# Last two tiles of a mixture-of-experts layer outside the loop, their logits placed on chip

## Chip, cores, metric

One core of a Trainium2 chip. The metric is the device time of one execution in microseconds (us), lower is better.

## What is computed

Sliding-window attention over 4 x 768 tokens (8 heads of 64), then two layers of experts over the same 3,072 rows of 512 numbers. Both have 8 experts, each a 512 x 1024 and a 1024 x 512 matrix. They differ in who goes where:

```python
# first layer: each token to its own best expert
logits = x @ w_gate + modality_bias[modality_id]
e_idx = np.argmax(logits, axis=1)
h = np.maximum(x[mask] @ w1[e], 0.0)
out[mask] = gate_w[mask, None] * (h @ w2[e])
# second layer: greedy over all (token, expert) pairs, 384 tokens an expert
order = np.argsort(-(x @ w_gate).flatten())
...
if assigned[tok] >= 0 or counts[e] >= cap: continue
```

So the second layer can assign nothing before the logits of all 3,072 rows of the first layer's output are known.

## The kernel before

**First layer.** The tokens are sorted by expert into tiles of 128, at least 24 and at most `MAXT` = 31 of them; how many there are is known only on the chip. DVE (VectorE) computes tables in `build_slots` (line 1296): `idx`, the token of each place of each tile; `tab`, per tile its group (`T_GRP`), the parity of its weight buffer (`T_PAR`), whether weights are to be split at it (`T_SPLIT`), and the number of tiles less 3 (`T_N`). `table_ready` releases SP's, ScalarE's and TensorE's weight work.

Each tile runs through these steps, written out as a queue by hand on each engine:

- GpSimd `gather` (576): the rows of x of tile i, by indirect DMA, into `xg`; `scatter` (585): `y` with its 8 logits back to `y_rows` in memory (columns 512 to 519 are the logits). There is one `y`; it is written again only when its scatter has landed.
- TensorE `step1(i)` (817): `up(i)` half 0 (12 matmuls), `transpose_h(i-1)` (8 transposes), `up(i)` half 1 (12), `transpose_x(i+1)` (4), `down(i-1)` (24 matmuls, into bank 5).
- ScalarE `step` (1073): `h_hi(i-1)` (copies the transposed hidden values rounded, in two halves, into `hh`), two `relu(i)`, `x_hi(i+1)`.
- VectorE `step` (1406): `h_lo(i-1)` (line 1393, two halves: the rest that the rounding left, into `hl`), logits 5 to 7 of tile i-2, `x_lo(i+1)`, then, when `down(i-1)` is done, `y` (line 1418), two copies of gates, logits 0 to 4 of tile i-1 (line 1404, `second_logits`). `down(i)` on TensorE waits for `h_lo(i)`. Each value times weight product is three matmuls (high by high, high by low, low by high).

Tiles 0 to 2 are written out. Then each engine has a loop of `MAXT - 3` = 28 turns, with a condition inside: turn k does tile k + 3, if k is below the number of tiles less 3; `split_next(i)` behind a tile reads `T_SPLIT` from `tab` (lines 1094, 1446). The unused turns come last. Behind the loop stand the last `transpose_h` and `down`, the last `y`, its 8 logits and the last two scatters.

```python
with dve.Fori(0, MAXT - 3) as k:          # 1462
    with dve.If(k < tiles.k):             # 1463
        i = Index(k, 3)
        step(0, i)
        split_next(i)
step(0, tiles, cur=False)
```

**Between the layers.** SP waits until all scatters have landed and loads the 3,072 x 8 logits into `l2` (lines 471, 472): 24 columns of tokens on 128 partitions. VectorE fills small tiles meanwhile (1475 to 1494) and waits for `l2_loaded`.

**Second layer.** Rounds `ph` = 0 to 6 each find the expert that fills first: a radix search for a threshold, 8 steps t of 4 bits. In a step VectorE compares (`compare`, 1511, operations `ge`), TensorE counts (848), VectorE marks full experts (1529), TensorE spreads (853), VectorE takes the digit (`next_digit`, 1532). At t = 1 and 2 `finite` (1483) changes thresholds that would be read as NaN or infinity: three chained VectorE operations. From round 1 on, TensorE's matmuls of the experts already filled (`hidden` 889, `outward` 902) stand between the steps of the search, and VectorE's low parts too; `pick_early` (1625) and GpSimd's `pick_late` build the list of an expert's rows, which `gather_second` reads from `y_rows`.

**Attention** comes first; GpSimd prepares keys there (`key_spans`, 511) and constants, and stores 128 zero rows behind x (571).

Of the kernel before, what the change touches and what calls it, by code (L numbers as in the profile page):

```python
# [15 lines left out]
P = 128  # L16
# [11 lines left out]
TC = N // P  # L28
# [30 lines left out]
SOON = 5  # L59
# [45 lines left out]
def val(x):  # L105

    if not isinstance(x, Index):
        return x
    k = x.k if x.m == 1 else x.k * x.m
    return k + x.c if x.c else k  # L110


def two_layers_of_experts(nc, queries, k, v_win, modality_id, w_gate, modality_bias, w1, w2,
                          w_gate2, w1b, w2b, out):
    ctx = ExitStack()
    with ctx:
# [35 lines left out]
        tab = sb("tab", [P, 6, 32], I32)  # L152
        T_PAR, T_GRP, T_SPLIT, T_EID, T_N = range(5)
# [4 lines left out]
        gidx = sb("gidx", [P, 1], I32)  # L158
        sidx = sb("sidx", [P, 1], I32)
        eids = sb("eids", [P, E], I32)  # L160
# [12 lines left out]
        first.close()  # L173

        second = ExitStack()
        sc = lambda name, shape, dt=F32: second.enter_context(nc.sbuf_tensor(name, shape, dt))
        xh2 = sc("xh2", [P, KC, CAP], F32R)
        xl2 = sc("xl2", [P, KC, CAP], F32R)
# [181 lines left out]
        down_done, y_done = two("down_done"), two("y_done")  # L360
        gate_loaded, l2_out = sem("gate_loaded"), sem("l2_out")
        l2_loaded = sem("l2_loaded")
        dve_chain2 = sem("dve_chain2")
# [124 lines left out]
        def _(pool):  # L488
# [81 lines left out]
            g.nop().then_inc(const_ready, 1)  # L570
            pool.dma_start(x_d[N:N + P, :], zrow[:, :]).then_inc(pad_stored, 16)
            for m in range(3, B * HP):
                key_spans(m)
                spread_means(m)
# [9 lines left out]

            def scatter(st, i):
# [6 lines left out]
                pool.indirect_dma_start(out=dst[:, :], out_offset=bass.IndirectOffsetOnAxis(ap=sidx[:, 0:1], axis=0),  # L592
                                        in_=y[:, 0:w], in_offset=None).then_inc(scattered[st], 16)

            for stored in x_stored:
                pool.wait_ge(stored, 16 * (B + 1))
            pool.wait_ge(pad_stored, 16)
            pool.wait_ge(idx_ready, 1)
            gather(0, 0)
# [5 lines left out]
            tiles = Index(pool.value_load(tab[0:1, T_N, 0:1], min_val=NT - 3, max_val=MAXT - 3), 3)  # L605
            with pool.Fori(0, MAXT - 3) as k:
                with pool.If(k < tiles.k):
# [4 lines left out]
            chain.start(base + 2 * (tiles - 3))  # L612
            scatter(0, tiles - 2)
            scatter(0, tiles - 1)
            base = base + 2 * tiles - 4
            def gather_second(r, t):
# [37 lines left out]
        def _(pe):  # L654
# [117 lines left out]

            def product(ps, lhs, rhs, n):

                for c in range(n):
                    for t, (a, b) in enumerate(((0, 0), (0, 1), (1, 0))):
                        last = mm(ps, lhs[a][:, c, :], rhs[b](c), start=c == 0 and t == 0, stop=c == n - 1 and t == 2)  # L777
                return last

# [24 lines left out]

            def down(st, i, g, par):
                pe.wait_ge(hlo_done[st], val(2 * i + 2))
                pe.wait_ge(wlo_done[st], val((W1U + W2U) * (g + 1)))
                pe.wait_ge(y_done[st], val(i))
                s_ = bass.ds(par, 1) if not isinstance(par, int) else slice(par, par + 1)
                rhs = [lambda c, w=w: w[:, s_, c, :].rearrange("p o f -> p (o f)") for w in (w2h, w2l)]  # L810
                product(bank[5][:, :], (hh, hl), rhs, FC).then_inc(down_done[st], 1)

# [24 lines left out]
            tiles = Index(pe.value_load(tab[0:1, T_N, 0:1], min_val=NT - 3, max_val=MAXT - 3), 3)  # L837
            with pe.Fori(0, MAXT - 3) as k:
                with pe.If(k < tiles.k):
                    step1(Index(k, 3))  # L840
            step1(tiles, cur=False)


            def count(ph, t):
# [130 lines left out]
        def _(act):  # L975
# [132 lines left out]
            tiles = Index(act.value_load(tab[0:1, T_N, 0:1], min_val=NT - 3, max_val=MAXT - 3), 3)  # L1108
            with act.Fori(0, MAXT - 3) as k:
                with act.If(k < tiles.k):  # L1110
                    i = Index(k, 3)
                    step(0, i)
                    split_next(i)
            step(0, tiles, cur=False)

# [50 lines left out]
        def _(dve):  # L1166
# [129 lines left out]
            def build_slots(st):  # L1296
# [40 lines left out]
                if st == 0:  # L1337
# [57 lines left out]

            def second_logits(i, experts):
                if 0 in experts:
                    dve.wait_ge(y_done[0], val(i + 1))
                for e in experts:
                    if e >= 2:  # L1400
                        dve.wait_ge(l2_out, val(E * i + (e - 1)))
                    elif not isinstance(i, int) or i > 0:
                        dve.wait_ge(l2_out, val(E * i + (e - 1)))
                    stt(bank[6 + e % 2][:, :], y[:, 0:DM], 1.0, wg2[:, e, :], ALU.mult, ALU.mult, accum_out=y[:, DM + e:DM + e + 1]).then_inc(l2_out, 1)  # L1404

# [55 lines left out]
            tiles = Index(dve.value_load(tab[0:1, T_N, 0:1], min_val=NT - 3, max_val=MAXT - 3), 3)  # L1461
            with dve.Fori(0, MAXT - 3) as k:
                with dve.If(k < tiles.k):
                    i = Index(k, 3)
# [5 lines left out]
            base = base + 2 * (tiles - 3)  # L1470
            chain.start(base)


            chain = Chain(dve, dve_chain2)
            chain(vec.memset(owner[:, :], -1.0))
# [17 lines left out]
            for t in range(STEPS - 1, 3, -1):  # L1493
                chain(tt(digits[:, t, :], digits[:, t, :], digits[:, t - 1, :], ALU.bitwise_xor))
            dve.wait_ge(l2_loaded, 16)

            def prepare(ph):
# [13 lines left out]
            def compare(ph, t):  # L1511
                if t in (1, 2):
                    finite(thr[:, :])
# [243 lines left out]
```

## Time and profile before

| | |
|---|---|
| runs shown, us | 1064.84, 1066.01, 1074.94; median 1066.01 |
| profiled execution, us | 1066.68 (its span 1064.9) |
| granted TensorE clock, mean | 0.925 |
| TensorE busy | 84% of the span |
| attention | 0 to about 218 us |
| tables | to 242 us |
| first layer | 242 to 597 us |
| scatter, reload | to 604 us |
| second layer | 604 to 1065 us |

The profile is of one execution. PE is TensorE, DVE VectorE, ACT ScalarE, POOL GpSimd; a `q` behind a name (DVEq, PEldq) marks what the engine's sequencer does itself: register operations, loads of a register, branches. In brackets stands the engine's idle time before an instruction and what ended it; "issue" is idle time in which it waited for nothing that the profile shows. `x13` is the number of instructions in a row. Line numbers are those of the kernel before.

### The profile page before, as it was taken

The numbers are of one execution on the slowest core, as the hardware profiler recorded it, in microseconds if no ns is written. First come the engines' busy times: TensorE is split into PE (matmuls) and PEld (weight loads), VectorE is DVE, ScalarE is ACT, GpSimd is POOL, SyncE is SP. The second block draws the span as 40 slices with busy tenths as digits, with TensorE's granted clock in tenths as the row PEclk, the third lists the DMA queues.
The fourth block names the chain that finished last, engine by engine and source line by source line (L and its number), as shares of the span: only waits on it lengthen the run. The fifth ranks groups of instructions, "written<-read, shape, count | busy, mean of one in ns | idle before, by whom it ended". The sixth has DMA issues, their size and how long they took to land.

```text
span 1064.9 us, 21948 instructions
## 1 busy us (share of the span) xinstructions
PE 898.2 (84%) x7342; PEld 733.7 (69%) x7343; DVE 681.6 (64%) x1998; ACT 305.5 (29%) x626; POOL 285.1 (27%) x390
## 2 busy tenths in 40 slices
PE   4899999915899999999996233999898989998995
PEld 3787878714688888888885122868686867687884
DVE  5757576575666666666665567777777768674440
ACT  2544454505322212222221003223232322223330
POOL 5733344101012111111220005050515151414501
PEclk9999999956899999999998655999999999999998
DMA  9676675915011111111110123414141414155100
GB/s 195 122 160 135 133 153 100 280 50 185 11 51 40 50 40 40 40 40 40 40 50 20 24 71 119 159 51 169 50 169 54 165 61 159 61 204 172 32 29 30
DMA packets 45631, 99.94 MB, mean 94 GB/s; under 512 B 6736, under 2 KB 19072, under 8 KB 45440
## 3 DMA queue, kind: packets, MB, share of 16 engines
q1 hardware_dynamic: 26816, 61.63, 19.8%
q0 software_dynamic: 8064, 26.46, 7.9%
q10 hardware_dynamic: 10688, 11.01, 4.9%
q8 instruction: 39, 0.64, 0.2%
q14 instruction: 24, 0.20, 0.1%
HBM read 79.57 MB, written 19.51 MB: 93 GB/s over the span
## 4 chain that ended last, share of the span: by engine, by line
PE 69%; DVE 18%; issue 4%; POOL 3%; ACT 2%; DMA 2%; DVEq 0%; ACTq 0%; SPq 0%; POOLq 0%
PE bank L777 27%; PE bank L898 11%; PE bank L912 9%; PE bank L689 4%; PE bank L670 3%; PE bank L848 3%; DVE w_low L1649 2%; PE bank L730 2%; PE bank L707 2%; PE bank L801 2%; PE bank L679 2%; POOL slot_hot L635 2%; DVE xl L1653 1%; DVE ge L1517 1%; ACT xh L1042 1%
## 5 line engine op out<-in xcount | busy, mean ns | idle before, releaser
L1404 DVE SCALAR_TENSOR_TENSOR bank<-y,wg 128x512 f32<-128x512 f32 x200 | 132.0, 723 | 2.9
L635 POOL TENSOR_SCALAR slot_hot<-iota_l,mlo 128x128 bf16<-128x128 f32 x96 | 72.0, 766 | 214.7 <-DVE mlo L1622 214.7
L898 PE MATMUL bank<-xh,w_high 128*128 128x384 f32 x256 | 94.3, 368 | 16.1 <-DVE hl L1639 8.9
L777 PE MATMUL bank<-w_high,hh 128*128 x200 | 83.2, 416 | 13.2 <-DVE hl L1393 13.2
L777 PE MATMUL bank<-w_high,xh 128*128 x200 | 82.7, 414 | 10.7 <-DVE gates L1386 10.7
L592 POOL DMA_INDIRECT y_rows<-y,sidx x25 | 25.0, 998 | 243.2 <-DVE bank L1404 243.2
L898 PE MATMUL bank<-xh,w_low 128*128 128x384 f32 x256 | 88.1, 344 | 0.0
L898 PE MATMUL bank<-xl,w_high 128*128 128x384 f32 x256 | 87.9, 344 | 0.0
L1042 ACT ACTIVATE hh<-bank 128x512 fp32r<-128x512 f32 x50 | 27.1, 595 | 203.1 <-PE bank L801 203.1
L1418 DVE TENSOR_SCALAR y<-bank,gates 128x512 f32<-128x512 f32 x25 | 18.8, 751 | 101.1 <-PE bank L777 101.1
L912 PE MATMUL bank<-w_high,hh 128*128 128x512 f32 x192 | 82.3, 429 | 0.0
L1042 ACT ACTIVATE w_high<-w_landed 128x1024 fp32r<-128x1024 f32 x64 | 63.1, 1049 | 66.0 <-DMA w_landed<-in_moe_w 66.0
L777 PE MATMUL bank<-w_low,hh 128*128 x200 | 80.5, 403 | 0.0
L777 PE MATMUL bank<-w_high,hl 128*128 x200 | 80.3, 402 | 0.0
L777 PE MATMUL bank<-w_low,xh 128*128 x200 | 80.3, 402 | 0.0
L777 PE MATMUL bank<-w_high,xl 128*128 x200 | 80.2, 401 | 0.0
L1649 DVE TENSOR_TENSOR w_low<-w_landed,w_high 128x1024 fp32r<-128x1024 f32 x64 | 77.8, 1219 | 0.8
L848 PE MATMUL bank<-ge,cb 128*8 128x16 bf16 x1344 | 42.3, 170 | 41.7 <-DVE ge L1517 41.6
L912 PE MATMUL bank<-w_high,hl 128*128 128x512 f32 x192 | 75.7, 394 | 0.0
L912 PE MATMUL bank<-w_low,hh 128*128 128x512 f32 x192 | 75.5, 393 | 0.0
L848 PEld LDWEIGHTS bank<-ge,cb 128*8 128x8 bf16 x1344 | 36.2, 83 | 54.6 <-DVE ge L1517 50.8
L1118 ACT ACTIVATE hh<-bank 128x384 fp32r<-128x384 f32 x64 | 31.5, 492 | 140.2 <-PE bank L898 140.2
(285 smaller groups left out, 1932.5 us busy)
## 6 DMA issues: line engine op xcount, KB each, us to landing
w_landed<-in_moe_w SPq DMA_DIRECT2D x16, 2048.0 KB, 10.5
va<-in_v_win SPq DMA_DIRECT2D x16, 585.0 KB, 6.4
raw_w<-in_moe_w SPq DMA_DIRECT2D x4, 2048.0 KB, 11.3
k_raw<-in_k SPq DMA_DIRECT2D x16, 384.0 KB, 9.1
q_eye<-in_q ACTq DMA_DIRECT2D x16, 384.0 KB, 7.4
x_rows<-x ACTq DMA_DIRECT2D x12, 384.0 KB, 10.2
wg<-in_moe_w_gate SPq DMA_DIRECT2D x1, 2048.0 KB, 25.8
x_rows<-x SPq DMA_DIRECT2D x4, 387.0 KB, 7.2
```

Of the source, the lines that this page charges most:

```text
L592: pool.indirect_dma_start(out=dst[:, :], out_offset=bass.IndirectOffsetOnAxis(ap=sidx[:, 0:1], axis=0), in_=y[:, 0:w], in_offset=None).the ...
L635: last = g.tensor_scalar(slot_hot[:, j, :], iota_l[:, :], mlo[:, j:j + 1], None, ALU.is_equal)
L670: last = mm(bank[n % 2][QB * s_:QB * s_ + QB, PW * (2 * t + h):PW * (2 * t + h) + PW], qe[hp % 2][:, h, QB * j:QB * j + QB], kbt[hp % 2][: ...
L689: last = mm(bank[4 + (n + 1) % 2][WK:PW, MEAN0:MEAN0 + 2 * D], average[:, j, :], va[m % HP][0:WK, :, j, 0:D], start=j == 0, stop=j == NQ - 1)
L777: last = mm(ps, lhs[a][:, c, :], rhs[b](c), start=c == 0 and t == 0, stop=c == n - 1 and t == 2)
L848: last = mm(bank[7][0:E, 0:KSEARCH], cb[:, j, :], ge[:, j, :], start=j == 0, stop=j == TC - 1)
L898: last = mm(bank[fc % 2][:, 0:CAP], w[:, q % 2, c, f], a[:, c, :], start=c == 0 and t == 0, stop=c == KC - 1 and t == 2)
L912: last = mm(bank[2 + t % 2][:, :], a[:, c, rows], w[:, q % 2, c, :], start=c == 0 and n == 0, stop=c == FC - 1 and n == 2)
L1042: copy = lambda o, a: nc.scalar.activation(o, a, ACT.Copy)
L1118: nc.scalar.activation(hh2[:, fc, :], bank[fc % 2][:, 0:CAP], ACT.Relu).then_inc(hhigh_done, 1)
L1404: stt(bank[6 + e % 2][:, :], y[:, 0:DM], 1.0, wg2[:, e, :], ALU.mult, ALU.mult, accum_out=y[:, DM + e:DM + e + 1]).then_inc(l2_out, 1)
L1649: tt(low, whole, high.bitcast(F32), ALU.subtract).then_inc(low_done, 1)
```

## The change

1. A table row `T_TURN` gives each loop turn its tile: `max(0, k + tiles - MAXT)`. The loops have `MAXT - 4` = 27 turns, the unused ones come first, and a used turn reads its tile's number from the table. They now end with the last tile but one.
2. The end is written out on each engine. TensorE computes `down` of the last tile but one in two halves with `transpose_h` of the last between them, and `down` of the last into bank 4. ScalarE instead of VectorE writes the last two y, one of them into `y_last`.
3. SP loads `l2` when all but the last two tiles are stored. GpSimd has stored zeros in the logit columns in attention. The last two scatters wait for this load.
4. The logits of the last two tiles go into `l2` on chip: GpSimd makes two one-hots for each tile from its token numbers (`slot_lo` by partition, `slot_hi` by column), VectorE multiplies the logits with `slot_hi` (`placed`), two fp32 matmuls with `slot_lo` put them on their partitions (bank 5), VectorE adds them to `l2`.
5. `finite` is called at t = 2 alone, not at t = 1.
6. `pick_early` waits for all stored rows. `l2` lies at the start of the buffers that the two layers share, so its load waits for the last splits too.

```diff
@@ tables
+ chain(ts(ne8[:, 0:1], tend8[:, E - 1:E], -float(MAXT), None, ALU.add))
+ chain(ts(tab[:, T_TURN, :], iota_t[:, :], ne8[:, 0:1], 0.0, ALU.add, ALU.max))
@@ all engines
+ def turn_of(eng, k):
+     return eng.value_load(tab[0:1, T_TURN, bass.ds(k, 1)], min_val=0, max_val=MAXT - 5)
- with dve.Fori(0, MAXT - 3) as k:
-     with dve.If(k < tiles.k):
-         i = Index(k, 3)
+ with dve.Fori(0, MAXT - 4) as k:
+     with dve.If(k + tiles.k > MAXT - 4):
+         i = Index(turn_of(dve, k), 3)
@@ SP
- sp.wait_ge(scattered[0], val(16 * tiles))
+ sp.wait_ge(scattered[0], val(16 * (tiles - 2)))
+ sp.wait_ge(l2_cleared, 16)
+ sp.wait_ge(wlo_done[0], val((W1U + W2U) * Index(groups, 1)))
@@ GpSimd
+ pool.dma_start(y_d[0:N, DM:YW].rearrange("(j p) e -> p j e", p=P),
+                zrow[:, 0:TC * E].rearrange("p (j e) -> p j e", e=E)).then_inc(l2_cleared, 16)
...
+ scatter(0, tiles - 3)
+ pool.wait_ge(slots_known, 1)
+ for i in range(2):
+     g.tensor_scalar(slot_lo[i][:, :], iota_l[:, :], lastf[:, 0, i:i + 1], None, ALU.is_equal)
+     last = g.tensor_scalar(slot_hi[i][:, :], iota_j[:, :], lastf[:, 1, i:i + 1], None, ALU.is_equal)
+ last.then_inc(slots_known, 1)
+ pool.wait_ge(l2_loaded, 16)
  scatter(0, tiles - 2)
- scatter(0, tiles - 1)
+ scatter(0, tiles - 1, y_last)
+ pool.wait_ge(scattered[0], val(16 * tiles))
+ pool.sem_inc(rows_stored, 1)
@@ TensorE
- step1(tiles, cur=False)
+ up(0, tiles - 1, g, par, 0)
+ transpose_h(0, tiles - 2)
+ up(0, tiles - 1, g, par, 1)
+ down(0, tiles - 2, gp, pp, part=0)
+ transpose_h(0, tiles - 1)
+ down(0, tiles - 2, gp, pp, part=1)
+ down(0, tiles - 1, g, par, into=4)
+ pe.wait_ge(slots_known, 2)
+ for i in range(2):
+     pe.wait_ge(rows_placed, i + 1)
+     last = mm(bank[5][:, 0:TC * E], slot_lo[i][:, :], placed[i][:, :, :]..., start=i == 0, stop=i == 1)
+ last.then_inc(rows_spread, 1)
@@ ScalarE
- step(0, tiles, cur=False)
+ step(0, tiles - 1, nxt=False)
+ act.wait_ge(down_done[0], val(tiles - 1))
+ h_hi(0, tiles - 1)
+ act.wait_ge(scattered[0], val(16 * (tiles - 2)))
+ nc.scalar.activation(y[:, 0:DM], bank[5][:, :], ACT.Copy, scale=gates[:, 0:1]).then_inc(y_done[0], 1)
+ act.wait_ge(down_done[0], val(tiles))
+ nc.scalar.activation(y_last[:, 0:DM], bank[4][:, :], ACT.Copy, scale=gates[:, 1:2]).then_inc(y_done[0], 1)
@@ VectorE
- step(0, tiles, cur=False)
- second_logits(tiles - 1, range(SOON, E))
+ h_lo(0, tiles - 2)
+ second_logits(tiles - 3, range(SOON, E))
+ (five small operations: lastidx, lastf from idx of the last two tiles), slots_known
+ h_lo(0, tiles - 1)
+ dve.wait_ge(slots_known, 2)
+ for n, rows in enumerate((y, y_last)):
+     second_logits(tiles - 2 + n, range(E), rows)
+     dve.wait_ge(l2_out, val(E * (tiles - 1 + n)))
+     tt(placed[n][:, :, :], rows[:, DM:YW].unsqueeze(1)..., slot_hi[n][:, :].unsqueeze(2)..., ALU.mult).then_inc(rows_placed, 1)
  (small fills, lines 1475 to 1494)
  dve.wait_ge(l2_loaded, 16)
+ dve.wait_ge(rows_spread, 1)
+ chain(tt(l2[:, :, :], l2[:, :, :], bank[5][:, 0:TC * E]..., ALU.add))
@@ search
-                 if t in (1, 2):
+                 if t == 2:
                      finite(thr[:, :])
...
  def pick_early(r):
+     dve.wait_ge(rows_stored, 1)
```

## Rows read from the trace of the kernel before

**Rows 1.** The page: busy us (share of the span) x instructions.

```profile
PE 898.2 (84%) x7342; PEld 733.7 (69%) x7343; DVE 681.6 (64%) x1998; ACT 305.5 (29%) x626; POOL 285.1 (27%) x390
```

**Rows 2.** Timeline (start us, us, engine, line) of turns 1, 2 and 24.

```profile
287.44 1.29 DVE L1393 TENSOR_TENSOR hl<-bank,hh 128x512 fp32r<-128x512 f32 x2
...
289.14 0.60 PE L784 MATMUL bank<-ident,xg 128*128 128x128 f32 x4
289.49 0.48 PE L777 MATMUL bank<-w_high,hh 128*128 x1
...
295.17 0.40 PE L777 MATMUL bank<-w_high,xh 128*128 x1
...
300.51 1.29 DVE L1393 TENSOR_TENSOR hl<-bank,hh 128x512 fp32r<-128x512 f32 x2 [0.55 <-issue]
...
302.14 0.49 PE L777 MATMUL bank<-w_high,hh 128*128 x1
...
565.31 1.29 DVE L1393 TENSOR_TENSOR hl<-bank,hh 128x512 fp32r<-128x512 f32 x2 [0.30 <-issue]
...
566.94 0.49 PE L777 MATMUL bank<-w_high,hh 128*128 x1
```

**Rows 3.** Chain of waits (start us, us, what), end of the first layer.

```profile
559.96 3.03 PE bank L777 x13
...
576.46 0.32 DVEq L1446
...
577.10 0.06 DVEq L1446
...
577.73 0.06 DVEq L1463
...
581.11 0.06 DVEq L1463
```

**Rows 4.** TensorE's sequencer, lines 791 (290 to 296 us) and 838 (560 to 570): ns, then starts.

```profile
L791 PEldq FUSED_REGOPS  x1: 42/42/42, 293.7 to 293.7; - x1
...
L838 PEldq ALU_OP  x2: 32/34/36, 568.8 to 569.5; - x2
```

**Rows 5.** Timeline of the first layer's end, all engines.

```profile
574.40 1.08 ACT L1042 ACTIVATE hh<-bank 128x512 fp32r<-128x512 f32 x2 [6.61 <-PE bank L801]
...
583.26 0.79 PE L777 MATMUL bank<-w_high,hh 128*128 x1 [8.46 <-DVE hl L1393]
...
590.93 0.75 DVE L1418 TENSOR_SCALAR y<-bank,gates 128x512 f32<-128x512 f32 x1 [6.05 <-PE bank L777]
...
597.04 0.08 DVE L1475 MEMSET owner<- 128x24 f32 x1
...
599.10 0.80 DVE L1494 TENSOR_TENSOR digits<-digits 128x16 int32<-128x16 int32 x4
604.30 0.06 DVE L1656 MEMSET mids<- 128x2 f32 x1 [4.39 <-DMA l<-y_rows]
```

**Rows 6.** Timeline of TensorE, its longest wait in the loop's first turns.

```profile
274.67 0.79 PE L777 MATMUL bank<-w_high,hh 128*128 x1 [4.75 <-DVE hl L1393]
```

**Rows 7.** Windows: us, PE, PEld, DVE, ACT, POOL busy, granted clock, DMA share, GB/s.

```profile
274.70:279.80 5.10, 5.10 (x12) 4.08 (x13) 0.27 (x2) 0.00 (x0) 1.36 (x3) 0.51 0.18 52
...
680.00:735.00 55.00, 50.50 (x482) 40.57 (x482) 41.59 (x145) 15.29 (x23) 16.99 (x18) 1.00 0.34 121
```

**Rows 8.** Timeline of the search's step t = 1 in the third round.

```profile
693.55 0.35 DVE L1485 TENSOR_SCALAR thm<-thr 128x16 int32<-128x16 int32 x1
694.51 0.63 DVE L1517 TENSOR_TENSOR ge<-smx,thr 128x192 bf16<-128x192 f32 x2
...
694.92 0.76 PE L848 MATMUL bank<-ge,cb 128*8 128x16 bf16 x24 [1.20 <-DVE ge L1517]
```

**Rows 9.** Timeline of GpSimd in attention.

```profile
7.11 1.64 POOL L509 DMA_DIRECT2D mid<-in_moe_modality_id  x1 [0.71 <-POOL k_raw L507]
...
48.35 0.66 POOL L521 COPY k_bias<-ksum 64x576 f32<-64x576 f32 x1 [2.34 <-DVE ksum L1186]
```

More of the change, by code:

```diff
@@ L152, in two_layers_of_experts @@
         tab = sb("tab", [P, 6, 32], I32)
-        T_PAR, T_GRP, T_SPLIT, T_EID, T_N = range(5)
+        T_PAR, T_GRP, T_SPLIT, T_EID, T_N, T_TURN = range(6)
         one_row = sb("one_row", [P, E * TC])
@@ L173, in two_layers_of_experts @@
         first.close()
+        closing = ExitStack()
+        sd = lambda name, shape, dt=F32: closing.enter_context(nc.sbuf_tensor(name, shape, dt))
+        sd("below_hid", [P, KC * F + FC * DM + YW + 2 * KC * P])
+        y_last = sd("y_last", [P, YW])
+        closing.close()
+        closing = ExitStack()
+        closing.enter_context(nc.sbuf_tensor("below_slot_lo", [P, TC * E], F32))
+        slot_lo = [closing.enter_context(nc.sbuf_tensor(f"slot_lo{i}", [P, P], F32)) for i in range(2)]
+        slot_hi = [closing.enter_context(nc.sbuf_tensor(f"slot_hi{i}", [P, TC], F32)) for i in range(2)]
+        placed = [closing.enter_context(nc.sbuf_tensor(f"placed{i}", [P, TC, E], F32)) for i in range(2)]
+        closing.close()
         second = ExitStack()
         sc = lambda name, shape, dt=F32: second.enter_context(nc.sbuf_tensor(name, shape, dt))
+        l2 = sc("l2", [P, TC, E])
         xh2 = sc("xh2", [P, KC, CAP], F32R)
@@ L583, in gather, with scatter @@
                                         ).then_inc(gathered[st], 16)
-            def scatter(st, i):
+            def scatter(st, i, rows=None):
                 if not isinstance(i, int) or i > 0:
@@ L605, in _ @@
             tiles = Index(pool.value_load(tab[0:1, T_N, 0:1], min_val=NT - 3, max_val=MAXT - 3), 3)
-            with pool.Fori(0, MAXT - 3) as k:
-                with pool.If(k < tiles.k):
-                    i = Index(k, 3)
+            with pool.Fori(0, MAXT - 4) as k:
+                with pool.If(k + tiles.k > MAXT - 4):
+                    i = Index(turn_of(pool, k), 3)
                     chain.start(base + 2 * (i - 3))
@@ L611, in _ @@
                     scatter(0, i - 2)
-            chain.start(base + 2 * (tiles - 3))
+            chain.start(base + 2 * (tiles - 4))
+            scatter(0, tiles - 3)
[5 more added lines that the diff above has]
+            pool.wait_ge(l2_loaded, 16)
             scatter(0, tiles - 2)
-            scatter(0, tiles - 1)
-            base = base + 2 * tiles - 4
+            scatter(0, tiles - 1, y_last)
+            pool.wait_ge(scattered[0], val(16 * tiles))
+            pool.sem_inc(rows_stored, 1)
             def gather_second(r, t):
@@ L771, in build_slots, with product @@
                 last.then_inc(slots_done, 1)
-            def product(ps, lhs, rhs, n):
-                for c in range(n):
+            last_mm = [None]
+            def product(ps, lhs, rhs, n, part=None):
+                for c in range(n) if part is None else range(n // 2 * part, n // 2 * part + n // 2):
                     for t, (a, b) in enumerate(((0, 0), (0, 1), (1, 0))):
-                        last = mm(ps, lhs[a][:, c, :], rhs[b](c), start=c == 0 and t == 0, stop=c == n - 1 and t == 2)
-                return last
+                        last_mm[0] = mm(ps, lhs[a][:, c, :], rhs[b](c), start=c == 0 and t == 0, stop=c == n - 1 and t == 2)
+                return last_mm[0]
             def transpose_x(st, i):
@@ L803, in transpose_h, with down @@
                         last.then_inc(hT_done[st], 1)
[L805 to L808, printed above, removed]
+            def down(st, i, g, par, into=5, part=None):
+                if part != 1:
+                    pe.wait_ge(hlo_done[st], val(2 * i + 2))
+                    pe.wait_ge(wlo_done[st], val((W1U + W2U) * (g + 1)))
+                    if into == 5:
+                        pe.wait_ge(y_done[st], val(i))
                 s_ = bass.ds(par, 1) if not isinstance(par, int) else slice(par, par + 1)
                 rhs = [lambda c, w=w: w[:, s_, c, :].rearrange("p o f -> p (o f)") for w in (w2h, w2l)]
-                product(bank[5][:, :], (hh, hl), rhs, FC).then_inc(down_done[st], 1)
+                product(bank[into][:, :], (hh, hl), rhs, FC, part)
+                if part != 0:
+                    last_mm[0].then_inc(down_done[st], 1)
             def group_of(i):
@@ L837, in _ @@
             tiles = Index(pe.value_load(tab[0:1, T_N, 0:1], min_val=NT - 3, max_val=MAXT - 3), 3)
-            with pe.Fori(0, MAXT - 3) as k:
-                with pe.If(k < tiles.k):
-                    step1(Index(k, 3))
-            step1(tiles, cur=False)
+            with pe.Fori(0, MAXT - 4) as k:
+                with pe.If(k + tiles.k > MAXT - 4):
+                    step1(Index(turn_of(pe, k), 3))
+            g, par = group_of(tiles - 1)
+            up(0, tiles - 1, g, par, 0)
+            transpose_h(0, tiles - 2)
+            up(0, tiles - 1, g, par, 1)
+            gp, pp = group_of(tiles - 2)
+            down(0, tiles - 2, gp, pp, part=0)
+            transpose_h(0, tiles - 1)
+            down(0, tiles - 2, gp, pp, part=1)
+            g, par = group_of(tiles - 1)
+            down(0, tiles - 1, g, par, into=4)
+            pe.wait_ge(slots_known, 2)
+            for i in range(2):
+                pe.wait_ge(rows_placed, i + 1)
+                last = mm(bank[5][:, 0:TC * E], slot_lo[i][:, :], placed[i][:, :, :].rearrange("p j e -> p (j e)"), start=i == 0, stop=i == 1)
+            last.then_inc(rows_spread, 1)
             def count(ph, t):
@@ L1467, in _ @@
                     split_next(i)
-            step(0, tiles, cur=False)
-            second_logits(tiles - 1, range(SOON, E))
-            base = base + 2 * (tiles - 3)
-            chain.start(base)
+            h_lo(0, tiles - 2)
+            second_logits(tiles - 3, range(SOON, E))
             chain = Chain(dve, dve_chain2)
+            chain(vec.tensor_copy(lastidx[:, 0, :], idx[:, bass.ds(val(tiles - 2), 2)]))
+            chain(ts(lastidx[:, 1, :], lastidx[:, 0, :], P - 1, None, ALU.bitwise_and))
+            chain(ts(lastidx[:, 2, :], lastidx[:, 0, :], 7, None, ALU.logical_shift_right))
+            chain(vec.tensor_copy(lastf[:, 0, :], lastidx[:, 1, :]))
+            chain(vec.tensor_copy(lastf[:, 1, :], lastidx[:, 2, :]))
+            vec.nop().then_inc(slots_known, 1)
+            h_lo(0, tiles - 1)
[3 more added lines that the diff above has]
+                dve.wait_ge(l2_out, val(E * (tiles - 1 + n)))
+                tt(placed[n][:, :, :], rows[:, DM:YW].unsqueeze(1).to_broadcast([P, TC, E]), slot_hi[n][:, :].unsqueeze(2).to_broadcast([P, TC, E]),
+                   ALU.mult).then_inc(rows_placed, 1)
             chain(vec.memset(owner[:, :], -1.0))
```

22 lines of the change are left out of this document (14 added, 8 removed).

## Prediction

> **What bounds the kernel now.** I read the page first: TensorE is busy for 84% of the span [rows 1], so the question in each stage is what it waits for. Then I read the timeline of single turns of the first layer's loop, the chain of waits with the register work of the sequencers in it, the timeline of the first layer's end, the windows with the granted clock, and the search's first steps.
>
> In the loop TensorE looks like the bound: it has no idle time worth a row. The timeline says more. Where VectorE's `h_lo` is early, the four transposes of `transpose_x` take 0.35 us and `down` follows (289.14 to 289.49); `h_lo` had ended at 288.73, 0.76 us before. In the next turn `h_lo` ends at 300.51 + 1.29 = 301.80 and `down` starts at 302.14; in the last it ends at 566.60 and `down` starts at 566.94 [rows 2]. Both times the distance is 0.34 us. So in steady state `down` starts when `h_lo` lets it, about 0.1 us later than TensorE could. The ring is: `down` ends, y, five logits, loop control, `h_lo`, `down`. There is no slack in it for VectorE: what is added to VectorE's loop control lengthens each tile one for one. The 0.30 us idle before `h_lo`, put down to "issue", is that control [rows 2].
>
> At the end of the first layer the waits are in series: `down` of the last tile starts 8.46 us after TensorE's transposes; VectorE computes y and 8 logits from 590.93 to 597.04; then come scatter and reload, for which VectorE waits 4.39 us until 604.30 [rows 5].
>
> **The change part by part**, in the profiled execution (span 1064.9, its time 1066.68 us). There are 25 tiles (200 logit operations, 8 a tile), so 6 turns are unused, before as after.
>
> *Table, +0.4 (0 to 0.6).* Two more small chained operations before `table_ready`; four such take 0.80 us [rows 5].
>
> *The turn's number, +14.0.* Each of the 21 used turns now reads its number from `tab` behind the `If`, on every engine. The nearest row is VectorE's read of `T_SPLIT`: load at 576.46, its branch at 577.10, 0.64 us for the load and the register work on it [rows 3]. With one addition more in the condition I take 0.70 (0.55 to 0.80: the load with half the register work, or a leading address operation too). On VectorE it stands between the last logits and `h_lo`, in the ring: 20 turns x 0.70 = 14.0 (11 to 16); the 21st is in the entry below. ScalarE and GpSimd are busy for 29% and 27% of the span [rows 1] and wait for the others in each turn; there it is hidden. TensorE's sequencer is ready with `up` at 293.7 and the matmul starts at 295.17, 1.5 us of lead [rows 2, 4], more than one read.
>
> The Trainium skill ("Runtime: NRT & Kernel Launch", Instruction fetch mechanics) gives about 200 ns for a register load. By it alone this term would be 20 x 0.2 = 4.0 us and the whole 10 us lower; the row above, with the register work behind the load, goes the other way, and I go by the row.
>
> *Unused turns first, +5.5.* On VectorE a skipped turn costs (581.11 - 577.73) / 5 = 0.68 us, six of them 4.1 [rows 3]. Added with the read to the `h_lo` that started at 300.51, it starts at 305.3, and `down` at 306.9 instead of 302.14: +4.8. TensorE pays too: its skipped turn is 0.7 to 0.75 (568.8, 569.5) [rows 4]; 6 x 0.75 + 0.8 for the read, less 1.5 of lead, leave it idle for 3.8 us before `up(3)`. After an idle time of 4.75 us it ran 12 matmuls at a granted clock of 0.51, the lower of its two levels, in 5.1 us [rows 6, 7], against 2.8 us at the upper one (13 in 3.03 us [rows 3]): 2.3 more. So `up(3)` starts at 299.0, and 5.1 + 0.7 + 2.8 + 0.4 later, at 308.0, `down(2)`: +5.9. I take 5.5 (4.3 to 7.0). Nothing covers this: one turn later all is as before.
>
> *The end, -11.1.* Count from the last tile's `up` at 559.96 [rows 3]; the other times are in [rows 5]. Now: `down(23)` can start at +7.0 as before [rows 2], its first half takes 2.8, `transpose_h(24)` 0.7 (twice the 0.35 of four transposes), the second half 2.8 and the end of the last matmul 0.2: +13.5. Only then may ScalarE overwrite `hh`: `h_hi` 0.54 for its first half (1.08 for both), `h_lo` 1.3, 0.34 to the matmul: `down(24)` at +15.7, where it was at 583.26 = +23.3. VectorE is free for this: the skipped turns that held it are gone, y is ScalarE's, and logits(23) come behind. TensorE idles 2.4 us, and may fall to the low clock; so I leave `down(24)` at the 7.65 us it took (583.26 to 590.93), a slow start included: +23.4. The copy of y and eight logits as from 590.93 to 597.04, 6.1, the placing product 0.4: +29.9. Behind it stand VectorE's small operations, 597.04 to 599.90 = 2.9 us, which were covered by the reload and now are on the path; they cover the two fp32 matmuls. Then the addition 0.4: search starts at +33.2, against 604.30 = +44.3. Gain 11.1 (9.0, if the placing work costs 2 us more than its neighbours; 13.4, if the clock does not fall: 5.6 for 24 matmuls). Late next is the last tile's own `down`. Logits(23), over 5 us, fit under it. The reload waits only for tile 22's scatter, and the 4.39 us for which it held VectorE fall long before it is needed; the two late scatters end far ahead of `pick_early` of the next round. GpSimd's four one-hots come when it has nothing to do.
>
> *Clearing DMA, 0 (0 to 1).* GpSimd issues 3,072 pieces; the like one took it 1.64 us. It waits 2.34 us for a block maximum right behind the place [rows 9], which hides it; the bytes are 96 KB.
>
> *`finite` at t = 1, -6.4.* Three chained VectorE operations fewer in each of 7 rounds. In the first, 3 x 0.2 = 0.6. In the other six they take 0.96 (693.55 to 694.51), and TensorE waits 1.20 us for what follows, longer than the saving [rows 8]: 6 x 0.96 = 5.8. This holds as long as no later wait takes it back; I bound it at 4.0 and 7.0.
>
> Sum: 0.4 + 14.0 + 5.5 - 11.1 + 0 - 6.4 = +2.4, so 1069.1 for an execution like the profiled one. The median of the runs shown, 1066.01, is 0.7 under that execution: 1068.4. A measurement of this kernel can tell about 1% (10.7 us) from no change. All ends together give -5.1 and +11.6 (the clearing included); the likeliest case's own range is 1061 to 1078.
>
> **The rivals.**
> *The read is hidden.* If the sequencer could read ahead of the branch, or the ring had slack, the 14 us fall away and the entry loses 0.7: 1068.4 - 14.7 = 1053.7. For it: TensorE shows no idle time. Against it: `down` starts 0.34 us behind `h_lo`, whatever the transposes take, and VectorE's idle before `h_lo` is 0.55 where control was longer and 0.30 where it was shorter, with `down` moving along [rows 2]. 12%.
> *The clock falls in the loop.* The new idle time of TensorE, about 0.8 us in each tile of 13.3, might bring the low clock back in each turn. At the 2.3 us that such a stretch costs [rows 3, 7], 20 turns cost 46: 1114. It decides from the granted clock in the loop: below 0.95 it is at work. Against it: the second layer keeps 1.00 with waits of 1.20 us in it [rows 7, 8]. 5%; that it strikes in some turns, 5% more.
> *The saved search steps come back late.* If each round of the second layer waits again for VectorE's other work or the landed weights, -6.4 becomes -0.6: 1074. For it: VectorE also computes the low parts and the lists of that stage. Against it: the 1.20 us are TensorE's own idle time, and at t = 1 only VectorE is waited for. 13%.
> The forecast has 65%.
>
> **How the numbers follow.** Time: 1068.4. The hidden read gives faster by over 1% (under 1055.3), if not all, and some of the rest lies in an end gain that I underrate: 16%. Slower by over 1% (over 1076.7) are the clock cases and the top of the forecast's own range: 12%. 72% are within 1%. The range of 8 in 10 runs from 1057, half of the read hidden with a good end, to 1077.
>
> **What would show it.** In the changed profile: period of a tile 13.3 us (now 566.94 - 302.14 over 21 tiles, 12.61) and VectorE's idle before `h_lo` near 1.0; a load of `tab` behind the loop's `If`; at tile 3 a gap of some 4 us on TensorE and a granted clock near 0.5 behind it; `down` of the last tile starting some 2.4 us after TensorE's previous matmul; search starting 33 us after the last `up`; no `thm` operation at t = 1 and the wait of 1.20 us down to 0.2. A period of 12.6 makes the first rival right. A search that starts later than +36 makes the end term wrong.

## The result and the profile after

The changed kernel takes 1076.10 us (median of 20 runs, 1067.64 to 1080.36), the kernel before 1068.76 us beside it (20 runs, 1064.23 to 1075.91). The medians lie 7.3 us apart; the ratio is 1.0058, 95% interval 1.0036 to 1.0080, so the change costs about 6.2 us (3.8 to 8.6). The forecast was +2.4, a difference that a measurement to 1% cannot tell from none. The absolute time is 0.9 us inside the upper end of the forecast range (1077), also because the kernel before took 2.8 us more here than in the runs shown (1066.01). The profiled execution took 1079.64 us (span 1077.9), so single profiles differ by more (+13.0) than the medians; which part of that is chance is the first thing to find out.

The page's busy times, which answer to [rows 1], say little: TensorE 84%, as before.

```profile
PE 907.8 (84%) x7342; PEld 737.5 (68%) x7343; DVE 675.6 (63%) x1981; ACT 305.9 (28%) x627; POOL 290.6 (27%) x394
```

The timeline of two turns of the loop, to be read against [rows 2]: VectorE idles 1.04 us before `h_lo`, where it was 0.30, and now TensorE too has an idle time in every turn, 0.58 us, put down to `h_lo`. The distance from the end of `h_lo` to `down` is 0.35 us, as it was.

```profile
329.66 1.29 DVE L1456 TENSOR_TENSOR hl<-bank,hh 128x512 fp32r<-128x512 f32 x2 [1.04 <-issue]
...
331.30 0.50 PE L812 MATMUL bank<-w_high,hh 128*128 x1 [0.58 <-DVE hl L1456]
...
343.01 1.29 DVE L1456 TENSOR_TENSOR hl<-bank,hh 128x512 fp32r<-128x512 f32 x2 [1.03 <-issue]
...
344.65 0.49 PE L812 MATMUL bank<-w_high,hh 128*128 x1 [0.59 <-DVE hl L1456]
```

The chain of waits in the same turn shows what fills the idle time: behind the read of `T_SPLIT` (1509, as [rows 3] had it) a second one, of the turn's number (417).

```profile
327.48 0.31 DVEq L1509
...
328.85 0.06 DVEq L417
328.94 0.30 DVEq L417
329.28 0.19 DVEq L417
329.66 0.07 DVE hl L1456
```

The entry into the loop (timeline of TensorE, then a window with busy times of PE, PEld, DVE, ACT, POOL, the granted clock, DMA share, GB/s). TensorE waits 4.17 us and then runs at a mean granted clock of 0.67, part of the stretch at the lower of its two levels, as in [rows 7].

```profile
309.45 0.49 PE L812 MATMUL bank<-w_high,xh 128*128 x1 [4.17 <-issue]
```

```profile
309.40:314.60 5.20, 5.15 (x19) 4.17 (x20) 1.26 (x4) 0.07 (x1) 0.00 (x0) 0.67 0.04 16
330.00:590.00 260.00, 248.46 (x1169) 199.62 (x1168) 160.64 (x447) 51.68 (x97) 46.44 (x78) 1.00 0.12 40
```

The second window is the loop: the clock stays at 1.00 there.

The end, first the last tile's `up` in TensorE's timeline, then the chain of waits, which answer to [rows 3, 5]. `down(24)` runs from 605.78, the last `placed` follows at 619.36, the addition to `l2` at 622.40, and the search starts at 622.83 behind VectorE's small operations.

```profile
590.28 0.39 PE L812 MATMUL bank<-w_high,xh 128*128 x1
```

```profile
594.11 5.80 PE bank L812 x24
599.90 0.87 PE bank L836 x8
600.78 2.81 PE bank L812 x12
603.61 0.61 ACT hh L1096
...
604.85 0.69 DVE hl L1456
...
605.78 7.41 PE bank L812 x24
613.22 0.70 ACT y_last L1175
...
619.36 0.36 DVE placed L1546
```

```profile
622.40 0.35 DVE L1571 TENSOR_TENSOR l<-l,bank 128x192 f32<-128x192 f32 x1
622.83 0.06 DVE L1733 MEMSET mids<- 128x2 f32 x1
```

To see where the rest went I cut the profile of every run at the same marks, all on VectorE's timeline: the operation on the first layer's logits (`lg`) for the last of attention's four batches, the last write of `tab`, `h_lo` of tiles 0, 2 and 22, and the search's first `smx`. "A tile" is the mean distance of two `h_lo` from tile 3 to tile 22. Differences in us, one profile a kernel:

| kernel (clearing DMA?) | start to `lg` | to `tab` | to `h_lo(0)` | (0) to (2) | a tile | (22) to search | search to end |
|---|---|---|---|---|---|---|---|
| before | 215.03 | 27.00 | 31.00 | 27.48 | 12.608 | 51.68 | 460.5 |
| after (yes) | 220.59 | 27.46 | 35.69 | 32.57 | 13.331 | 39.98 | 455.0 |
| clear_only (yes) | 218.69 | 26.98 | 31.09 | 26.67 | 12.608 | 52.75 | 461.1 |
| clear_again (yes) | 215.88 | 27.00 | 35.72 | 27.58 | 12.611 | 51.68 | 459.2 |
| clear_x4 (four) | 220.73 | 26.97 | 31.13 | 27.01 | 12.611 | 51.53 | 462.4 |
| finite_only | 214.52 | 26.99 | 35.79 | 26.69 | 12.612 | 52.76 | 455.0 |
| turns_only | 219.08 | 27.45 | 30.98 | 33.25 | 13.333 | 48.38 | 460.1 |
| after_clear_late (yes) | 222.96 | 27.44 | 31.04 | 33.38 | 13.332 | 39.93 | 456.7 |
| after_arith (yes) | 218.84 | 27.46 | 35.77 | 32.50 | 12.682 | 38.44 | 457.2 |
| after_dve_arith (yes) | 218.15 | 27.46 | 31.28 | 32.48 | 12.684 | 39.96 | 454.7 |
| after_soon4 (yes) | 219.23 | 27.47 | 35.94 | 33.08 | 12.683 | 39.79 | 454.3 |
| after_unused_last (yes) | 217.65 | 26.97 | 35.95 | 26.75 | 12.624 | 42.51 | 456.4 |
| after_split_loop (yes) | 220.59 | 26.98 | 31.22 | 26.53 | 12.574 | 42.98 | 456.6 |
| after_nested (yes) | 217.09 | 26.99 | 31.06 | 27.05 | 12.618 | 40.47 | 456.3 |

Read down a column: a term of the change shows in each kernel that has it and in none that hasn't. Two columns don't follow the edits in this way. Up to `lg` everything from 214.5 to 223.0 occurs (how far the clearing is in it, see the sum below). Tables to `h_lo(0)` has two values, 31 and 36, and one and the same program (clear_only, clear_again) shows both.

### The profile page after: what moved, and what is told of

It is laid out like the page before. It is cut to its first block, busy times and chain, and to the rows that moved or that the text cites. A ratio compares the mean times of both kernels' runs of the same rounds, so it can differ in the third digit from the quotient of the medians.

```text
span 1077.9 us, 22242 instructions
## 1 busy us (share of the span) xinstructions
PE 907.8 (84%) x7342; PEld 737.5 (68%) x7343; DVE 675.6 (63%) x1981; ACT 305.9 (28%) x627; POOL 290.6 (27%) x394
## 4 chain that ended last, share of the span: by engine, by line
PE 53%; DVE 23%; issue 10%; POOL 4%; DVEq 3%; ACT 3%; DMA 3%; ACTq 0%; SPq 0%; POOLq 0%
PE bank L812 16%; PE bank L952 11%; PE bank L966 8%; PE bank L722 3%; PE bank L703 3%; POOL slot_hot L668 3%; PE bank L902 2%; DVE w_low L1726 2%; DVE bank L1467 2%; PE bank L763 2%; DMA q_eye<-in_q 2%; PE bank L740 2%; PE bank L712 2%; DVE hl L1456 2%; DVE xl L1730 1%
## 5 line engine op out<-in xcount | busy, mean ns | idle before, releaser
L1467 DVE SCALAR_TENSOR_TENSOR bank<-y,wg 128x512 f32<-128x512 f32 x192 | 126.7, 723 | 2.7
L1096 ACT ACTIVATE hh<-bank 128x512 fp32r<-128x512 f32 x50 | 27.1, 595 | 222.2 <-PE bank L836 216.1
L703 PE MATMUL bank<-k_bias,q_eye 128*64 128x120 f32 x768 | 52.8, 282 | 19.8 <-DVE k_bias L1257 12.3
L1052 ACT ACTIVATE probs<-bank,nmax 128x120 f32<-128x120 f32 x192 | 53.3, 365 | 33.9 <-DVE nmax L1295 33.7
```

The source lines that it names most:

```text
L703: last = mm(bank[n % 2][QB * s_:QB * s_ + QB, PW * (2 * t + h):PW * (2 * t + h) + PW], qe[hp % 2][:, h, QB * j:QB * j + QB], kbt[hp % 2][: ...
L1052: last = nc.scalar.activation(probs[n % 3][:, a, :], bank[n % 2][:, PW * a:PW * a + PW], ACT.Exp, bias=nmax[n % 2][:, a:a + 1], scale=SCALE)
L1096: copy = lambda o, a: nc.scalar.activation(o, a, ACT.Copy)
L1467: stt(bank[6 + e % 2][:, :], rows[:, 0:DM], 1.0, wg2[:, e, :], ALU.mult, ALU.mult, accum_out=rows[:, DM + e:DM + e + 1]).then_inc(l2_out, 1)
```

## The experiments

**1. The clearing DMA alone: clear_only, clear_again, clear_x4.**

```diff
@@ before
+ pool.dma_start(y_d[0:N, DM:YW]..., zrow[:, 0:TC * E]...).then_inc(l2_cleared, 16)
...
  pool.wait_ge(pad_stored, 16)
+ pool.wait_ge(l2_cleared, 16)
@@ clear_x4: four of them
+ for c0 in (DM, 0, 128, 256):
```

> The kernel before with one thing added: GpSimd's DMA of zeros into the 3,072 x 8 logit columns in attention, and the wait for it ahead of the first gather. Theory C (the small pieces of this DMA stand in the way of the loads of q, and so cost the changed kernel what it lost over the forecast): +3 to +6 us, TensorE waiting some 10 us at 50 us for a load of q that the kernel before does not wait for, and the tables ready 3 to 6 us later than 242.2. Theory L (the clearing is covered; the 6 us by which the tables came later in the changed kernel's profile are the luck of that one execution): 0 to +1 us in the medians.

Measured: 1.0034 (1.0002 to 1.0066), +3.6 us.

> The kernel before with four such clearing DMAs in a row in attention (the logit columns and three other groups of 8 columns, of 3,072 pieces each), and the wait for all of them. If one costs 3.6 us by its traffic or by GpSimd's time (theory C; clear_only had 1.0034, 1.0002 to 1.0066), four cost about 14 us: 1.013. If its cost is hidden and the 3.6 us were the spread of attention between executions (theory L): 0 to +3 us, and less than 1.004; here GpSimd is held for some 4 times 1.5 us, so that a small cost by its queue alone would be 3 to 4 us.

Measured: 1.0082 (1.0054 to 1.0111), +8.8 us.

> The same kernel as clear_only once more, for the one term that is still open: one clearing DMA in attention was 1.0034 (1.0002 to 1.0066), four of them 1.0082 (1.0054 to 1.0111). If one costs about a quarter of four or more, by its traffic: 1.002 to 1.0035 again. If the first interval was luck and four cost only by GpSimd's queue: 0.999 to 1.001. In the profile, if it costs by the engines that wait, TensorE's waits in attention for GpSimd or for loads of q are over 2 us longer in sum than in kernels without it; if not, the start of the tables varies with the granted clock of attention alone.

Measured: 0.9977 (0.9948 to 1.0007), -2.5 us. The two intervals of the same kernel overlap only from 1.0002 to 1.0007; together they say +0.5 us, give or take some 2. That one profile of the changed kernel had a wait for `q_eye` in the chain, which first made me suspect the clearing, is no evidence: the kernel before has such a wait too (chains of waits, after first):

```profile
50.75 10.40 DMA q_eye<-in_q
```

```profile
98.01 11.43 DMA q_eye<-in_q
```

Four DMAs do cost, and the timeline of GpSimd shows one way in clear_x4: the issuing takes 5.67 us and the key bias follows without any idle time; it was 0.93 us of idle time with one DMA and 2.34 without [rows 9].

```profile
42.28 5.67 POOL L574 DMA_DIRECT2D y_rows<-zrow  x4
50.89 0.66 POOL L522 COPY k_bias<-ksum 64x576 f32<-64x576 f32 x1
```

```profile
42.53 1.44 POOL L573 DMA_DIRECT2D y_rows<-zrow  x1
47.76 0.66 POOL L522 COPY k_bias<-ksum 64x576 f32<-64x576 f32 x1 [0.93 <-DVE ksum L1190]
```

The first fence is clear_x4, the second clear_only. TensorE's waits for GpSimd's queue in attention, from the view of waits (times, then the longest):

```profile
PE bank L675 <- POOLq L523: 8.9, 7, 3.7
```

```profile
PE bank L674 <- POOLq L523: 5.7, 8, 1.3
```

8.9 us is clear_x4, 5.7 us clear_again, and turns_only, without any clearing, has 5.7 as well (the kernel before 4.2). So the issue of one DMA lies in GpSimd's idle time, as forecast, and in these two measurements its cost is not told from nothing. A quarter of the four, 2.2 us, would fit them as well.

**2. The same program, two values: the second gather.** GpSimd's copy of 128 numbers for the gather of tile 1, timeline of clear_only and of clear_again:

```profile
254.07 1.22 DVE L1384 TENSOR_TENSOR w_low<-raw_w,w_high 128x1024 fp32r<-128x1024 f32 x1
...
254.22 1.11 POOL L581 COPY gidx<-idx 128x1 int32<-128x1 int32 x1 [12.11 <-DVE gates L1390]
```

```profile
251.29 4.62 DVE L1384 TENSOR_TENSOR w_low<-raw_w,w_high 128x1024 fp32r<-128x1024 f32 x4
...
251.44 4.52 POOL L581 COPY gidx<-idx 128x1 int32<-128x1 int32 x1 [12.12 <-DVE gates L1390]
```

The same copy for tile 0, with nothing beside it, took 0.19 us in both. Here it starts 0.15 us behind the first of VectorE's four `w_low` operations in both, and ends 0.04 us behind one of them: behind the first in clear_only (254.07 + 1.22 = 255.29; the copy 255.33), behind the last in clear_again (251.29 + 4.62 = 255.91; the copy 255.95). All 14 profiles have the one or the other. What decides between them no run shows. It moves `h_lo(0)` by 4.7 us (31 or 36 in the table, in exactly the profiles with 1.1 and 4.5): 3.4 us are the copy's, the rest comes behind it, where TensorE has waited longer for the gathered rows (timelines, clear_only first):

```profile
262.47 0.66 PE L788 MATMUL bank<-ident,xg 128*128 128x128 f32 x4 [0.67 <-DMA xg<-x_rows,gidx]
```

```profile
263.86 1.11 PE L788 MATMUL bank<-ident,xg 128*128 128x128 f32 x4 [4.92 <-DMA xg<-x_rows,gidx]
```

The profile of after had drawn 4.5, that of before 1.1. That is 4.7 of the 13.0 us between the two profiles; a later `lg` is 5.6 more.

**3. `finite` alone: finite_only.**

```diff
-                if t in (1, 2):
+                if t == 2:
```

> The kernel before with finite at t = 2 alone. Forecast's term: -6.4 us (-4 to -7), TensorE's wait at t = 1 down from 1.20 to about 0.2 us in the rounds 1 to 6. The rival by which the saved steps come back late: -0.6 us, with a longer wait elsewhere in the same round.

Measured: 0.9964 (0.9932 to 0.9996), -3.8 us. By the view of waits for the second layer TensorE waits 35.7 us for `ge` instead of 41.6, and the waits for low parts stay (9.0 after 8.9, 7.2 and 7.2). A little comes back late: the wait for the lists' `slot_hot` is 3.7 instead of 3.2 us, in all nine kernels without `finite` at t = 1. The first fence is before, the second finite_only.

```profile
PE bank L848 <- DVE ge L1517: 41.6, 23, 16.2
...
PE bank L885 <- POOL slot_hot L635: 3.2, 3, 1.5
```

```profile
PE bank L848 <- DVE ge L1517: 35.7, 21, 16.3
...
PE bank L885 <- POOL slot_hot L635: 3.7, 3, 1.5
```

The mean of search to end is 460.7 in the five kernels with `finite` at t = 1 and 455.8 in the nine without: -4.9. The profile of finite_only alone has 455.0, -5.7 from that mean.

**4. The turns alone: turns_only.** The kernel before with `T_TURN`, `If(k + tiles.k > MAXT - 4)` and the read; end and number of turns as before.

> The kernel before with nothing but the row T_TURN, the unused turns first and the turn's number read from the table, still 28 turns and the end as it was. By the terms: +0.4 (table), 22 turns x 0.72 = +15.8, of which one stands in the entry, entry +5.1 in place of skipped turns at the end, which now leave VectorE 4 us earlier. At the end the last down waited 8.46 us for VectorE's h_lo, so the skipped turns were on the path there and moving them gives about 4 back: +16 to +18 us in all. If the skipped turns at the end were covered by other work: +21. Period of a tile 13.3 us.

Measured: 1.0140 (1.0091 to 1.0188), +15.0 us. The period is 13.333, the entry 33.25, and (22) to search 48.38 against 51.5 to 52.8: the skipped turns at the old end had been on the path.

**5. The number computed, not read: after_arith and after_dve_arith.**

```diff
@@ after, all four engines (after_dve_arith: VectorE alone)
- return eng.value_load(tab[0:1, T_TURN, bass.ds(k, 1)], min_val=0, max_val=MAXT - 5)
+ e = (k + n + (35 - MAXT)) % 32
+ return eng.snap(nc.s_assert_within(e, 0, MAXT - 5, ...))
```

> The changed kernel with the turn's number computed in registers (k + tiles + constant, modulo 32) instead of read from tab. If it is the load from memory with the register work behind it that costs 0.72 us a turn: period back to 12.6 to 12.8 us, -11 to -14 us against the changed kernel, which is 0.989 to 0.995 of the kernel before. If it is the longer condition and the addresses that follow from a turn's number that is no longer the loop's own register: the period stays over 13.1 and the time within 3 us of the changed kernel.

Measured: 0.9932 (0.9904 to 0.9960), -7.3 us, so some 13 us under the changed kernel, by one expression. The period is 12.682. VectorE's idle time before `h_lo` (timeline) is back at 0.40, and TensorE waits for nothing:

```profile
327.27 1.29 DVE L1457 TENSOR_TENSOR hl<-bank,hh 128x512 fp32r<-128x512 f32 x2 [0.40 <-issue]
...
328.90 0.49 PE L813 MATMUL bank<-w_high,hh 128*128 x1
```

> The changed kernel in which VectorE alone computes the turn's number in registers, and TensorE, ScalarE and GpSimd read it from tab as before. The forecast had their reads hidden: then this equals after_arith (period 12.68, 0.993 of the kernel before; entry, h_lo(0) to h_lo(2), about 32.5 or a little more, since TensorE's read stands there too). If one of the others' reads is in the ring as well, the period lies between 12.8 and 13.33.

Measured: 0.9955 (0.9923 to 0.9987), the period 12.684. So the reads on TensorE, ScalarE and GpSimd are hidden in the steady state, and VectorE's alone costs: 0.65 us of the 0.72 a turn. The instructions of line 417 in after (ns, shortest, median, longest) show that they take as long there:

```profile
L417 ACTq TENSOR_LOAD <-tab x21: 275/282/287, 303.9 to 571.9; - x21
...
L417 PEldq TENSOR_LOAD <-tab x21: 301/303/311, 306.7 to 573.8; - x21
...
L417 DVEq TENSOR_LOAD <-tab x21: 300/308/317, 315.6 to 582.2; - x21
```

Only the first turn of the loop (`h_lo(2)` to `h_lo(3)`) is longer, 13.71 us against 12.70 in after_arith (after_soon4 has 13.74); no run shows why.

**6. Other work out of the ring: after_soon4.**

```diff
- SOON = 5
+ SOON = 4
```

> The changed kernel with 4 logits instead of 5 between y and h_lo; the fifth (0.65 us on VectorE) comes behind h_lo, where VectorE later idles 3.8 us for the next down. Ring theory (all that VectorE does between y and h_lo counts one for one while TensorE has idle time): TensorE has about 0.7 us to spare in a turn of 13.33, so the period falls to 12.68 and the time by 0.65 x 21 = 13 us, to 0.994 of the kernel before. If x_lo, which now comes 0.65 us later, or the scatter, which waits for the last logit, holds TensorE or y in its turn, the period stays between 12.9 and 13.33, and the chain names it.

Measured: 0.9960 (0.9929 to 0.9990), the period 12.683, 0.65 less. The read is still there; a logit has made room for it. The timeline of the turn has a new releaser for y, the scatter. `h_lo`'s 1.03 us are put down to ScalarE's `hh`, but `hh` had ended at 404.75, 0.84 us before `h_lo` started; this is the loop's control with the read, as in after:

```profile
400.54 0.75 DVE L1481 TENSOR_SCALAR y<-bank,gates 128x512 f32<-128x512 f32 x1 [3.13 <-DMA y_rows<-y,sidx]
...
403.66 1.09 ACT L1096 ACTIVATE hh<-bank 128x512 fp32r<-128x512 f32 x2 [8.37 <-PE bank L836]
...
405.59 1.29 DVE L1456 TENSOR_TENSOR hl<-bank,hh 128x512 fp32r<-128x512 f32 x2 [1.03 <-ACT hh L1096]
```

TensorE has no idle time any more (busy for all of the 120 us from 400 to 520): the turn can't get much shorter this way. The period fits the ring: 12.608 + 0.72 - 0.65 = 12.68.

**7. The clearing later: after_clear_late.** The DMA behind the last `key_spans`.

> The changed kernel with the clearing DMA issued at the end of GpSimd's work in attention (behind the last key_spans) instead of between the third and the fourth. Theory C: -3 to -4 us against the changed kernel, so a ratio of 1.002 to the kernel before. Theory L: within 1 us of the changed kernel, 1.005 to 1.007.

Measured: 1.0044 (1.0025 to 1.0064). Inconclusive: it lies between the two theories, 1.5 us below the changed kernel's ratio, with intervals that overlap.

**8. Unused turns last: after_unused_last, after_split_loop, after_nested.**

```diff
@@ after_unused_last
- with eng.If(k + tiles.k > MAXT - 4):
-     i = Index(turn_of(eng, k), 3)
+ with eng.If(k < tiles.k - 1):
+     i = Index(k, 3)
@@ after_nested
+ with eng.Fori(0, NT - 3) as k:
+     with eng.If(k < tiles.k - 1):
...
+ with eng.If(tiles.k - 1 > NT - 3):
+     with eng.Fori(NT - 3, MAXT - 4) as k:
+         with eng.If(k < tiles.k - 1):
...
```

> The changed kernel with the unused turns last again, so no T_TURN and no read. Expected: table -0.5, read -14.4, entry -5.1 against the changed kernel; in return VectorE's 6 skipped turns (0.68 us each, 4.1 in all) stand ahead of h_lo of the last tile but one, whose down then starts up to 3.9 us later, and nothing covers that: sum -16 us, 1060 us, 0.991 of the kernel before, with 16 us from its h_lo to that of the tile before in place of 12.3. If the end has slack for the skipped turns: -20, 0.987. Attention and the first gather's luck can move a single profile by 5 us each.

Measured: 0.9898 (0.9868 to 0.9928), -10.9 us.

> after_unused_last with the first 20 turns, which are used whatever the tokens are (24 tiles at least), in a loop without a condition, and only the last 7 in a loop with one. If the condition and its branch cost VectorE 0.1 to 0.2 us in each turn and VectorE is in the ring: period 12.4 to 12.5 us, 2 to 4 us less than after_unused_last. If the distance of h_lo's is set by TensorE as soon as VectorE gains 0.1 us (the forecast had down 0.1 us later than TensorE could): period 12.5, -2 us. If a second copy of the turn's code costs its fetching: a longer first turn in each loop, and no gain.

Measured: 0.9914 (0.9881 to 0.9947), -9.2 us. The period falls by 0.05 us only, and the first turn of the loop (12.87 against 12.67) and the passage at its end (16.85 against 16.37) take most of that back: a miss for the idea that the condition is dear. Either the condition costs less than was thought, or TensorE's own work takes some 12.57 us a turn; no run tells which.

> after_unused_last with its loop in two parts, 21 turns, and 6 more as a whole behind one condition, so that with 25 tiles no turn is skipped but one condition passed (with more tiles it costs what it did). If a skipped turn costs VectorE 0.68 us on the path: 16.4 us from h_lo of tile 22 to that of tile 23 fall to 12.8 to 13.0, -3.5 us against after_unused_last (0.990), so 0.987 of the kernel before. If TensorE or the fetch of a second copy of the code is late there instead: less than 1.5 us.

Measured: 0.9850 (0.9802 to 0.9898), median 1054.84 us beside 1070.39: about 16 us faster than the kernel before. It has the best ratio of all, though with 5 executions its interval overlaps those of after_unused_last and after_split_loop. The timelines of VectorE, after_unused_last first, show the idle time of the skipped turns before `h_lo` of the last tile but one go:

```profile
576.22 1.29 DVE L1450 TENSOR_TENSOR hl<-bank,hh 128x512 fp32r<-128x512 f32 x2 [4.08 <-issue]
```

```profile
567.44 1.29 DVE L1467 TENSOR_TENSOR hl<-bank,hh 128x512 fp32r<-128x512 f32 x2 [0.54 <-issue]
```

`h_lo(22)` to `h_lo(23)` falls from 16.37 to 12.85, -3.5 as expected. Of this 2.0 arrive at the search in these profiles, since `down(24)` took 7.4 us in after_nested and 5.9 in after_unused_last. The windows of that stretch (columns as above, the granted clock third from the end; after_nested first) show that TensorE's clock was lower in the one:

```profile
578.00:585.40 7.40, 7.40 (x26) 5.88 (x26) 5.31 (x17) 0.05 (x1) 1.24 (x2) 0.78 0.01 2
```

```profile
586.80:592.70 5.90, 5.90 (x26) 4.76 (x26) 5.28 (x17) 0.04 (x1) 0.37 (x2) 1.00 0.00 0
```

## Why the prediction was right, point by point

*The turn's number, +14.0.* Measured over 20 turns from `h_lo(2)` to `h_lo(22)`: (13.35 + 19 x 13.331) - (12.65 + 19 x 12.608) = +14.4, 0.72 a turn. The ring held (experiments 5 and 6), and the first rival, the hidden read, fell. By the trace's rows 0.31 us of it are the load and the rest is register work around it and the longer condition. The Trainium skill ("Runtime: NRT & Kernel Launch", Instruction fetch mechanics) has about 200 ns for a register load; the runs have 308 ns for the load alone and 0.72 us in all, and the measurement decides.

*Unused turns first, +5.5.* The column (0) to (2) has 27.1 in the five kernels with the old order and the old end, 32.9 in the six with the new: +5.8, with the gap on TensorE (4.17 us, forecast 3.8) and the low clock behind it. The low clock cost less than forecast: the 12 matmuls behind the gap took 4.60 us in the chain of waits, not 5.1, because the clock rose again on the way: from 313.4 on the matmuls start 0.23 us apart, before that 0.43.

```profile
309.45 4.60 PE bank L812 x12
```

*The end, -11.1.* Last `up` at 590.28 to the search at 622.83 is 32.55, forecast 33.2: -11.8. `down(24)` started 2.21 us after TensorE's previous matmul (forecast 2.4) and ran partly at the low level: 7.41 us, forecast 7.65 (by the rows, 590.93 - 583.26 is 7.67). Where the clock didn't fall (after_arith) the end is 1.5 us shorter, less than the bound of 2.3, which is itself too wide: 7.65 - 5.6 is 2.05. That it fell in the profile of after was even chance: of the eight profiles with the new end, all with 2.21 us of idle time there, five have 7.4 us and three 5.9.

*`finite`, -6.4.* The term that was sized too high, though inside its bounds: -4.9 in the columns, -5.7 in the profile of finite_only, -3.8 (-7.3 to -0.4) by its ratio. In the third round TensorE's wait of 1.20 us [rows 8] fell to 0.45, not to 0.2:

```profile
711.91 0.75 PE L902 MATMUL bank<-ge,cb 128*8 128x16 bf16 x24 [0.45 <-DVE ge L1593]
```

So 0.75 of the 0.96 us of three operations arrive there, and 0.5 us in all come back at `slot_hot`.

*Clearing DMA, 0 (0 to 1).* Not settled. GpSimd issues it in 1.44 us and its idle time covers that, as forecast. The time of the same kernel was +3.6 and -2.5 in two measurements; a cost of some 2 us is as good a reading of all runs as none (see the sum).

*Table, +0.4.* 0.46 in each of the kernels with it.

*Clock in the loop.* Didn't fall: 1.00 with 0.58 us of idle time in each turn.

*Sum.* 0.5 + 14.4 + 5.8 - 11.8 - 4.9 = +4.0, where the forecast had +2.4; 1.5 of the difference is `finite`. The ratio says +6.2 (3.8 to 8.6). The table says where to look for the 2.2 us between: ahead of `h_lo(0)`. For each of the eight kernels with the new end, add up its columns from `tab` on without the one to `h_lo(0)`, and compare with the kernel before: the time by its ratio is on average 2.8 us longer than that (from -0.5 in after_clear_late to +5.3 in after_soon4). Of the kernels on the old end, the two without a clearing DMA give +1.4 and -2.0, the two with one +2.8 and -1.2, clear_x4 +7.6. The column to `lg` agrees: on average 219.0 in the ten profiles with one clearing DMA and 216.2 in the three with none. A term of 2 to 3 us for each clearing DMA, where the forecast had 0, would fit all this. It is an estimate and not shown, since single profiles of one kernel differ there by 2.8 us (clear_only, clear_again) and only three have no clearing. How often the copy of experiment 2 waits long may also differ; 14 profiles are too few to tell.

That +2.4 lay near the result is in part luck: the forecast's terms of +19.9 and -17.5 us nearly cancel, and an error of a tenth in either sum would be nearly as large as the whole.

The sum is a gain of 16.7 us at the end and in the search, and a loss of 20.7 in the loop's new form. The end doesn't need that form: after_unused_last and after_nested keep the one and drop the other.

## What to carry to other kernels

Before a value that changes in every turn is put into a table, look at what stands between the last operation of one turn and the first of the next on the engine that closes the ring (the cycle of waits that sets the length of a turn). Here a load there cost 0.65 to 0.72 us, as much as a vector operation over 512 columns; register arithmetic a tenth of it; and the same load on engines with slack nothing in the steady state. A skipped turn cost VectorE 0.68 us at the start of the loop as at its end; one condition around them gave back 3.5 us at the loop's end. And take two profiles of the same program before reading a difference of one stage as the edit's.

## What the runs showed of the hardware

- GpSimd's copy of 128 x 1 numbers took 0.19 us alone. Started 0.15 us behind the first of four `w_low` operations of VectorE (128 x 1024, 1.22 us each), it ended 0.04 us behind the first of them (1.11 us, 8 of the 14 profiles) or behind the fourth (4.5 us, 6 of them), in the same program.
- A load of a register from on-chip memory took 0.28 us on ScalarE, 0.29 on GpSimd, 0.30 on TensorE, 0.31 on VectorE; with the register work around it VectorE lost 0.72 us a turn. The same number by an addition and a modulus lengthened the turn by 0.07.
- Behind the same idle time of 2.21 us on TensorE the granted clock was 0.78 in after_nested (24 matmuls in 7.4 us) and 1.00 in after_unused_last (5.9 us): with the same wait it fell in five of the eight profiles with the new end and not in the other three.
